# Banded attention on one core: both heads of a pair in one step, scores from split q and k, value products of 128 columns

## The reference, cut to what matters

```python
scores = (1 / sqrt(D)) * q @ k.T                     # D = 64, f32
keep = is_global | is_local                          # key < 8, or 0 <= rel < 96
bias = -slopes[h] * where(is_global & ~is_local, n_local, abs(rel))
a = softmax(where(keep, scores + bias, -1e9))
attn_out = a @ v                                     # then moe_ref, moe2_ref
```

## Time and profile before

| | us |
|---|---|
| Median of 3 runs (lowest, highest) | 1260.1 (1259.48, 1260.19) |
| Profiled execution | 1259.87 |
| Its span | 1258.2 |
| TensorE busy | 1060.5 (84%) |
| VectorE busy | 737.8 (59%) |
| ScalarE busy | 425.2 (34%) |

### The profile page before, as it was taken

One profiled execution on the slowest core, in us unless ns is written; L12 is line 12 of the kernel. 1 busy time (PEld: TensorE's weight loads), 2 busy tenths in 40 slices (PEclk: granted clock), 3 DMA queues, 4 the chain that ended last, 5 costly groups with the idle time before them and its releaser, 6 DMA issues.

```text
span 1258.2 us, 22559 instructions
## 1 busy us (share of the span) xinstructions
PE 1060.5 (84%) x6072; PEld 849.7 (68%) x6073; DVE 737.8 (59%) x2010; ACT 425.2 (34%) x885; POOL 193.1 (15%) x242
## 2 busy tenths in 40 slices
PE   8999999999863999999999996122317999999995
PEld 5666666666652788888888885111216889998884
DVE  4555455455486658778878767555564455544441
ACT  3444444444343425443442442000001334433320
POOL 1212112121000111121112111100002032233310
PEclk8999999999986999999999998555556999999998
DMA  8343343533140614234343404000001444455300
GB/s 190 87 95 92 90 105 76 120 71 87 46 183 9 211 61 169 88 127 167 116 160 117 163 33 151 27 1 0 0 0 51 151 148 151 170 183 183 117 26 26
DMA packets 146017, 127.26 MB, mean 101 GB/s; under 512 B 102381, under 2 KB 114669, under 8 KB 145840
## 3 DMA queue, kind: packets, MB, share of 16 engines
q1 hardware_dynamic: 137168, 99.67, 26.5%
q0 software_dynamic: 8800, 27.01, 6.2%
HBM read 107.78 MB, written 20.71 MB: 102 GB/s over the span
## 4 chain that ended last, share of the span: by engine, by line
PE 71%; DVE 15%; issue 6%; DVEq 3%; ACT 1%; ACTq 1%; DMA 1%; POOL 0%; SPq 0%; POOLq 0%
PE ps_o L378 10%; PE ps_s L347 9%; PE ps_o L924 9%; PE ps_s L901 8%; PE ps_o L1293 7%; PE ps_s L1277 6%; PE ps_pT L1277 5%; PE ps_pT L361 5%; DVE product L1122 4%; PE ps_s L1293 3%; PE ps_t L1451 2%; PE ps_t L331 2%; PE ps_pT L912 1%; PE ps_t L733 1%; DVEq L1125 1%
## 5 line engine op out<-in xcount | busy, mean ns | idle before, releaser
L924 PE MATMUL ps_o<-w_split_parts,hs 128*128 x696 | 167.8, 397 | 10.3 <-ACT hs L1000 9.6
L901 PE MATMUL ps_s<-w_split_parts,xs 128*128 x696 | 168.0, 397 | 2.1 <-issue 1.1
L471 DVE CUSTOM_DVE_ANT_0 arena_p<-ps_s,arena_b 128x256 f32<-128x256 f32 (+1 forms) x192 | 77.0, 401 | 144.0 <-PE ps_s L347 142.6
L924 PEld LDWEIGHTS ps_o<-w_split_parts,hs 128*128 128x128 f32 x696 | 129.6, 189 | 38.1 <-issue 11.7
L1122 DVE SCALAR_TENSOR_TENSOR product<-y_sb,wg_all 128x512 bf16<-128x512 f32 x232 | 150.9, 688 | 6.2 <-ACT y_sb L1018 1.2
L901 PEld LDWEIGHTS ps_s<-w_split_parts,xs 128*128 128x128 f32 x696 | 130.1, 190 | 29.2 <-issue 3.1
L540 ACT ACTIVATE arena_p<-arena_p,min_s 128x256 f32<-128x256 f32 (+1 forms) x192 | 94.0, 490 | 104.8 <-DVE min_s L471 100.2
L347 PE MATMUL ps_s<-kT,qT 64*128 64x256 f32 (+1 forms) x384 | 128.7, 417 | 0.7 <-ACT qT L527 0.7
L378 PE MATMUL ps_o<-vn,arena_p 128*128 128x192 f32 x384 | 95.1, 330 | 1.4 <-DVE arena_p L481 1.4
L1293 PE MATMUL ps_o<-w_split_parts,hs 128*128 128x512 f32 x384 | 94.1, 397 | 0.0
L347 PEld LDWEIGHTS ps_s<-kT,qT 64*128 64x128 f32 x384 | 57.8, 188 | 40.7 <-issue 29.2
(11 more groups left out here) (261 smaller groups left out, 1652.9 us busy)
## 6 DMA issues: line engine op xcount, KB each, us to landing
raw<-in_moe_w SPq DMA_DIRECT2D x32, 2048.0 KB, 9.4
y_rows<-y_sb POOLq DMA_DIRECT2D x31, 256.0 KB
kn<-in_k SPq DMA_DIRECT2D x32, 192.0 KB, 3.4
qn<-in_q SPq DMA_DIRECT2D x32, 192.0 KB, 3.5
vn<-in_v SPq DMA_DIRECT2D x32, 192.0 KB, 2.8
x_rows<-arena_x SPq DMA_DIRECT2D x96, 64.0 KB, 1.6
va<-in_v SPq DMA_DIRECT2D x32, 120.0 KB, 2.6
wg_rows<-in_moe_w_gate SPq DMA_DIRECT2D x1, 2048.0 KB, 9.0
```

What stands on the lines that cost most here:

```text
L471: nc.vector.tensor_tensor_reduce(out=neg_s[:, n % slots, 0:w], in0=raw, in1=add, scale=1.0, scalar=HUGE, op0=ALU.add, op1=ALU.min, accum_o ...
L901: last = nc.tensor.matmul(ps_s[:, f, :], xs[:, a, c * P:(c + 1) * P], weights(par, w, cols), start=(n == 0), stop=(n == len(passes) - 1))
L924: last = nc.tensor.matmul(ps_o[:, 0, :], hs[:, a, c * P:(c + 1) * P], weights(par, 2 + w, slice(c * DM, (c + 1) * DM)), start=(n == 0), st ...
```

## The change

The banded and the dense form get functions of their own; only the banded one runs with these inputs. In it, a step is now one tile row of both heads, six a pair. Each score is the sum of three f32r products, of high and low parts: q and k are copied out of PSUM rounded to f32r by ScalarE (`high_qk`), and VectorE subtracts that copy from the bank for the low part (`low_qk`); `qk_kept` is now counted by VectorE, and a new semaphore, `qk_high`, passes from ScalarE to it. The three products of both heads alternate, and each head has its own bank; the fourth score bank is the second one of `ps_pT`, and both heads' turned probabilities share its first one. The first pair's three groups are turned into three banks. The value products have 128 columns, and both heads' results for three tiles share a bank of `ps_o`; a normalization covers three tiles of both heads, and stands ahead of the copy of that step, not behind it.

```diff
-VALUED = P + D
+ATT0 = 6
...
+            def score(it, s):
+                par, i = s // QT % 2, s % QT
+                if i == 0:
+                    pe.wait_ge(qk_kept, it * 6 + s // QT * 3 + 3)
+                pe.wait_ge(biased, it * 24 + 2 * s - 2 + ATT0)
+                a, w = KS * (i - 1) + GK if i else 0, width(i)
+                for n, (qa, ka) in enumerate(TERMS):          # ((0, 0), (0, 1), (1, 0))
+                    for hh in range(2):
+                        rows = slice(D * hh, D * hh + D)
+                        band = k_part[ka][rows, par].rearrange("p t c -> p (t c)")[:, a:a + w]
+                        last = nc.tensor.matmul(SCORE_BANKS[(2 * s + hh) % 4][:, 0:w], q_part[qa][rows, par, i * P:(i + 1) * P], band,
+                                                start=(n == 0), stop=(n == len(TERMS) - 1))
...
+            def turn_probs(it, s):
+                pe.wait_ge(exped, it * 24 + 2 * s + 2 + ATT0)
+                pe.wait_ge(p_kept, it * 12 + s + ATT0)
...
+            def value(it, s):
...
+                pe.wait_ge(p_kept, it * 12 + s + 1 + ATT0)
+                for hh in range(2):
+                    at = i % 3 * P + hh * D
...
+                        a = t * P + D * hh
+                        last = nc.tensor.matmul(ps_o[:, i // 3, at:at + P], probsT_b[:, s % STEPS_HELD, hh, c * P:(c + 1) * P],
+                                                tiles[:, par, a:a + P], start=(c == 0), stop=(c == len(parts) - 1))
...
+            def two_pairs(it, last_one):                      # TensorE
+                for s in range(STEPS2):
+                    if s + AHEAD < STEPS2 or not last_one:
+                        score(it, s + AHEAD)
+                    turn_probs(it, s)
+                    if s > 0:
+                        value(it, s - 1)
+                    if s % QT < 3 and not (last_one and s >= QT):
+                        turn(it * 2 + s // QT + 1, it + s // QT, 1 - s // QT, s % QT)
+                value(it, STEPS2 - 1)
...
+            def low_qk(pair, par, g):                         # VectorE
+                dve.wait_ge(qk_high, pair * 3 + g + 1)
...
+                if g == 0:
+                    nc.vector.tensor_tensor(kl[:, 0:4, 0:P], src, kh[:, 0:4, 0:P], ALU.subtract)
+                    last = nc.vector.tensor_tensor(kl[:, 0:QT - 1, P:KS], bank[:, 0:GK].unsqueeze(1).to_broadcast([P, QT - 1, GK]),
+                                                   kh[:, 0:QT - 1, P:KS], ALU.subtract)
+                elif g == 1:
+                    nc.vector.tensor_tensor(kl[:, 4:6, 0:P], src[:, 0:2], kh[:, 4:6, 0:P], ALU.subtract)
+                    last = nc.vector.scalar_tensor_tensor(ql[:, 0:2 * P], bank[:, 2 * P:4 * P], minus, qh[:, 0:2 * P],
+                                                          ALU.mult, ALU.subtract)
+                else:
+                    last = nc.vector.scalar_tensor_tensor(ql[:, 2 * P:6 * P], bank, minus, qh[:, 2 * P:6 * P],
+                                                          ALU.mult, ALU.subtract)
+                last.then_inc(qk_kept, 1)
...
+            def two_pairs(it, last_one):                      # VectorE
+                for s in range(STEPS2):
+                    if s + AHEAD < STEPS2 or not last_one:
+                        bias_scores(it, s + AHEAD)
+                    if s > 3 and s % 3 == 1:
+                        norm(it, s // 3 - 1)
+                    keep_turned(it, s)
+                    if 1 <= s % QT <= 3 and not (last_one and s >= QT):
+                        low_qk(it * 2 + s // QT + 1, 1 - s // QT, s % QT - 1)
+                norm(it, 3)
...
+            def two_pairs(it, last_one):                      # ScalarE
+                for s in range(STEPS2):
+                    exp(it, s)
+                    if s % QT in (2, 3, 4) and not (last_one and s >= QT):
+                        high_qk(it * 2 + s // QT + 1, 1 - s // QT, s % QT - 2)
```

More of the change, by code:

```diff
@@ L306, in apart, with parts_of, pe_dense @@
             eng.sem_inc(passed, 1)
[L309 to L315, removed]
+        def parts_of(i):
+            return [(vn, 0)] if i == 0 else [(va, i - 1), (vn, i)]
         LAST = PAIRS // 2 - 1
-        def pe_attention(pe, fast):
-            probs, probsT, slots = probs_of[fast], probsT_of[fast], SLOTS[fast]
+        TERMS = ((0, 0), (0, 1), (1, 0))
+        def pe_dense(pe):
             def turn(pair, nth, par, g):
@@ L398, in pe_attention, with turn_bank, width @@
                 score(0, n)
+            with pe.Fori(0, LAST) as it:
+                two_pairs(it, False)
+            two_pairs(LAST, True)
+        FIRST_TURNS = [ps_t[:], ps_o[:, 0, :], ps_o[:, 1, :]]
+        def turn_bank(pair, g):
+            return FIRST_TURNS[g] if isinstance(pair, int) and pair == 0 else ps_t[:]
+        SCORE_BANKS = [ps_s[:, 0, :], ps_s[:, 1, :], ps_s[:, 2, :], ps_pT[:, 1, :]]
+        STEPS2 = 2 * QT
+        def width(i):
+            return P if i == 0 else BAND
@@ L456, in bias_scores @@
                 dve.wait_ge(scored, it * 24 + n + 1)
-                dve.wait_ge(exped, it * 24 + n + 1 - slots + INIT)
+                dve.wait_ge(exped, it * 24 + n + 1 - SLOTS + ATT0)
                 apart(dve)
[L460 to L470, removed]
+                both = arena_b[:, (1 + hh) * NB_DENSE:(2 + hh) * NB_DENSE]
@@ L569, in make @@
                 if not first:
-                    pool.wait_ge(biased, pair * 12 - (12 if fast else 0) + INIT)
+                    pool.wait_ge(biased, pair * 12 - (12 if fast else 0) + ATT0)
                     apart(pool)
@@ L589, in pool_attention, with pool_banded, pool_dense, by_form @@
                     make(it, par, False)
[L591 removed]
+        def pool_banded(pool):
+            pool_attention(pool, True)
+        def pool_dense(pool):
+            pool_attention(pool, False)
+        def by_form(eng, banded, dense):
             eng.wait_ge(form_known, 1)
[L594 to L596 removed]
+            is_banded = eng.value_load(form_i[0:1, 0:1], min_val=0, max_val=1)
+            with eng.If(is_banded > 0):
+                banded(eng)
             with eng.Else():
[L598 removed]
+                dense(eng)
         def x_chunk(tile_i, c):
@@ L1762, in done @@
                 dve.drain()
-            for name, start in ((biased, INIT), (p_kept, INIT), (normed, NORM0)):
+            for name, start in ((biased, ATT0), (p_kept, ATT0), (normed, NORM0)):
                 dve.sem_inc(name, start)
```

223 lines of the change are left out of this document (157 added, 66 removed).

## The result

The changed kernel takes 1223.9 us (median of 4 runs, 1222.8 to 1227.6) against 1260.1: a ratio of 0.972, interval 0.970 to 0.974, 36 us less. The forecast was 1227, with 1208 to 1246 around it. The profiled execution took 1227.6, with a span of 1225.9, 32 us under the span before.

The account below looks back on a forecast made before the run. TensorE was taken to bound attention, with a new chain over VectorE after the change. Savings of 29 us over 15 pairs plus 5 in the last, less 1.4 at the beginning, made 33: 1260 to 1227 us, range 1208 to 1246.

Parts of the forecast that it names:

- Value products: Attention steps on TensorE: 128 columns in place of 192 take 0.22 us each, not 0.33; 0.88 a step against 1.32.
- The gap at each change of array shape: TensorE between score and turn: fixed 0.20 us; with the smaller gaps 0.34 us a step, now once for two heads.
- Six products: Both heads' f32r score products in a step: 0.54 us taken, weight loads queuing; ends 0.36 and 0.73.
- the third case: Rival, scores: both array halves run at once, loads too, 0.36 us for six products; 1215 us, chance 0.25.
- The chain over VectorE: q/k turns and next pair's score wait for VectorE's low parts: steps 1 to 3 last 3.68, 3.54, 3.01 us.
- The dearest wait: Step 7 of each loop pass: TensorE idle 2.5 us, from about 1.8 until its turn can start at 4.3.
- the fourth case: Rival, attention stage: new TensorE waits lower the clock; 1277 us at half the stage, 1325 at all; chance 0.08.
- a pair: Attention stage: one pair takes 18.2 us with the branch, against 20.16 before, at clock 1.00.

Follow-up runs that it names:

- the f32 kernel: Changed kernel with plain f32 scores, no low parts, and the normalization behind the copy: 1161.4 us, ratio 0.920 to the kernel before; 1185.7 with 192-column value products.
- one of two such moves: Changed kernel with VectorE making the low parts ahead of the copy of the turned probabilities: 1206.5 us.
- the other alone: Changed kernel with only the normalization moved behind the copy, the low parts behind both: 1222.8 us.
- both: Changed kernel with the low parts ahead of the copy and the normalization behind it: 1182.8 us.

## Why the prediction was right

- *Value products* at 0.22 us each: right. What they are worth depends on how much TensorE waits: 13 us in the change, 24 in the f32 kernel, 38 if it never waited. Nothing was said of the danger to the clock in a kernel without waits; the prediction weighed the clock only where TensorE stands still.
- *The gap at each change of array shape*, 0.20 us, once for both heads: agrees, but is not measured apart. What is measured is 0.64 us for both heads in plain f32, which is the 0.43 of one product and the 0.20, and 0.55 with the split.
- *Six products*: mis-sized. 0.54 was taken, 0.35 measured, if the gap is 0.20: not only the products but also the weight loads of the two halves run at once, the third case. By the prediction's own terms this is 12 us less than forecast (1215).
- *The chain over VectorE*: right in place and in size. At 0.36 for the scores the four steps shown were put at 4.64 (3.57 and a normalization), 3.43, 2.90 and about 2.0; measured 4.75, 3.98, 3.07 and 1.96 with a spell at half clock in the second and third, and 3.52, 2.94 for these two at full clock:

```profile
152.67 0.38 PE L435 MATMUL ps_s<-k_high,q_high 64*128 64x256 f32 x2
156.19 0.38 PE L435 MATMUL ps_s<-k_high,q_high 64*128 64x256 f32 x1
159.13 0.33 PE L435 MATMUL ps_s<-k_high,q_high 64*128 64x128 f32 x2 [0.84 <-DVE q_low L610]
```

  The dearest wait, in step 7, was forecast at 2.5 us and is 2.5.
- *What was left out*: the fourth normalization of a loop pass. It stands behind the last value product, VectorE waits 1.25 us for that, and the next pass's first biasing, copy and low part come later by it. In order of time, at full clock:

```profile
165.49 0.56 DVE L649 TENSOR_TENSOR arena_x<-ps_o,sums 128x384 f32 x1 [0.17 <-issue]
166.13 0.38 PE L435 MATMUL ps_s<-k_high,q_high 64*128 64x256 f32 x1
166.18 0.42 DVE L626 CUSTOM_DVE_ANT_0 arena_p<-ps_s,arena_b 128x256 f32<-128x256 f32 x1
169.70 0.44 PE L420 MATMUL ps_t<-ident,kn 128*128 128x128 f32 x2 [1.25 <-DVE k_low L603]
170.29 0.38 PE L435 MATMUL ps_s<-k_high,q_high 64*128 64x256 f32 x2
```

  Step 1 of the pass's first pair lasts 4.16 (166.13 to 170.29) instead of 3.57: 0.6, seven times, some 4 us.
- *The clock*: the fourth case came in small. From 22 to 304 us the trace has nine spells at half rate, 3.4 us each, as from 133.5:

```profile
130.00:133.20 3.20, 1.37 (x14) 0.98 (x10) 3.02 (x12) 2.74 (x10) 0.00 (x0) 1.00 0.89 205
133.20:136.60 3.40, 3.38 (x18) 2.83 (x19) 1.25 (x5) 1.45 (x5) 0.00 (x0) 0.55 0.37 107
140.00:180.00 40.00, 29.83 (x256) 24.85 (x255) 26.38 (x93) 17.90 (x66) 9.89 (x9) 1.00 0.41 95
```

  They come behind waits, but not behind each: from 140 to 180 the same waits left the clock at 1.00. In the steps shown a spell cost 0.6 us (3.98 and 3.07 against 3.52 and 2.94). All twelve steps of a loop pass, each at full clock, add up to 35.7 us; the seven passes took 256.4, from 22.82 to 279.18, some 7 us more than seven times that. It is little because a slower TensorE mostly shortens its own wait: the third turn waited for its low part in only 8 of 15 pairs. No run changed the clock alone.

So two errors cancel, and that the forecast of 1227 comes so close to 1224 is luck: 12 us too much for the scores, some 11 too little for the fourth normalization and the clock, 1226 in all (the traced execution took 1227.6). The same holds for a pair, 18.2 us forecast and 18.3 measured (256.4 for 14 pairs), with the clock at 0.95 and not at 1.00.

Which theory holds? Each in part. The narrower products are a third of the gain if taken last, and nearly all of it if taken first and the clock comes up; shared steps with scores at once give 23 us without them. What the change gives back, it gives back by the low parts on VectorE and their place in its order, not by more work on TensorE.

## What to carry to other kernels

Two products with 64 contraction rows in different halves of the array cost the time of one in this kernel, weight loads too, in f32 as in f32r; take that first, and only then ask whether splitting into cheaper products still pays, with its extra work on another engine counted where it stands in the queue. When an engine gets new work that another one waits for, put it ahead of everything in its program that nobody waits for yet, all of it: here one of two such moves gave 17 us, the other alone 1, both 41. After narrowing a product, look at the clock and at more than two or three runs: the kernel with 128 columns alone had 1228 and 1335 us among five. And two edits that shorten the same engine's work do not add up once that engine waits for another.

## What the runs showed of the hardware that was not expected

- The two halves of the array go through their products each on its own: with three products of one head ahead of three of the other in the program, both heads' first products start 0.02 us apart.
- Weight loads of the halves run at once too: both start at 124.72, and six loads and products take 0.35 us (0.55 less a gap of 0.20), where loads one behind the other would take 0.54 at the 0.09 of the earlier trace rows, an estimate.
- The clock can stay at half with TensorE working all the time: busy for 193.7 of 194.4 us, from 11.8 to 206.2, in the traced run with value products of 128 columns. With 192 columns it came up at 22.5 us and with 160 at 31. Five runs with 128 differ by 106 us. What decides it is open.
- Spells at half clock cost less than they look: nine of 3.4 us took some 7 us from the changed kernel, where TensorE waits anyway, and more where it had work to do (4.99 us for a step of 3.53).
- The Trainium skill, "TensorE: Matmul & The Clock Gate", section Part 3: Packing small matmuls, says that matmuls start and end in program order, without reordering. The trace with the heads in turn disagrees on the starts, with the 0.02 us above; the measurement decides.
